# A fused attention, gated feed-forward and token/channel mixing kernel: the first batch in three units of 192 tokens instead of two of 288

## The reference

```python
# 1: attention; heads 0-3 look at the last 32 keys, heads 4-7 at every 4th of the last 128
scores = where(mask, q @ k.T / 8, -1e9)          # softmax over keys, then @ v
x = attention.transpose(0, 2, 1, 3).reshape(4, 576, 512)
# 2: gated feed-forward with a shift by one token
xk = mu_k * x + (1 - mu_k) * x_prev;  xr = mu_r * x + (1 - mu_r) * x_prev
x = sigmoid(xr @ w_r) * (relu(xk @ w_k) ** 2 @ w_v)        # w_k 512x1024, w_v 1024x512
# 3: mixing
u = x + (relu(x.T @ w_tok1) @ w_tok2).T
out = u + relu(u @ w_ch1) @ w_ch2
```

## Time and profile before

| | |
|---|---|
| runs (3) | 782.77 us median, 782.66 to 783.21 |
| the profiled execution | 783.69 us, of which its span is 781.9 us |
| PE busy | 741.8 us, 95% of the span |
| DVE, ACT, POOL busy | 375.3, 256.7, 238.4 us |
| mean granted TensorE clock | 0.995 |

### The profile page before, as it was taken

How to read it: one execution, slowest core, us unless ns; L and a number is a source line. 1 busy time by engine, 2 the same in 40 slices (tenths; PEclk the granted TensorE clock), 3 DMA queues, 4 the chain that set the end, 5 groups by cost and what they waited for, 6 DMA issues and landing times.

```text
span 781.9 us, 15662 instructions
## 1 busy us (share of the span) xinstructions
PE 741.8 (95%) x6616; PEld 716.2 (92%) x6616; DVE 375.3 (48%) x594; ACT 256.7 (33%) x636; POOL 238.4 (30%) x245
## 2 busy tenths in 40 slices
PE   4778999999999999999999999999999999999997
PEld 3667999989898999989999999999999999999997
DVE  5737875757676675767674121521225111341211
ACT  2445354353535344353442111411123111241111
POOL 5848464564656455473407200000000000000000
PEclk9998999999999999999999999999999999999999
DMA  8912312302302212020180100210002100010001
GB/s 200 249 35 42 67 35 59 74 14 56 75 18 57 61 26 59 19 61 1 48 337 1 62 1 1 62 61 1 1 1 71 52 1 1 1 62 1 2 1 60
DMA packets 67797, 39.80 MB, mean 51 GB/s; under 512 B 55120, under 2 KB 59024, under 8 KB 67728
## 3 DMA queue, kind: packets, MB, share of 16 engines
q1 hardware_dynamic: 65583, 34.09, 16.7%
q0 software_dynamic: 1088, 4.72, 1.8%
q10 hardware_dynamic: 1056, 0.00, 0.1%
HBM read 29.36 MB, written 4.72 MB: 44 GB/s over the span
## 4 chain that ended last, share of the span: by engine, by line
PE 81%; POOL 8%; issue 3%; ACT 3%; DVE 3%; DMA 1%; ACTq 0%; DVEq 0%; SPq 0%; POOLq 0%
PE bank L605 13%; PE bank L606 12%; PE bank L607 12%; PE tq L605 5%; PE tq L606 5%; PE tq L607 5%; PE bank L529 3%; PE bank L1021 3%; PE bank L1020 3%; PE s L1021 3%; PE bank L1019 3%; PE s L1019 3%; PE s L1020 3%; PE bank L500 3%; PE s L425 2%
## 5 line engine op out<-in xcount | busy, mean ns | idle before, releaser
L605 PE MATMUL bank<-xk_hi,WK_hi 128*128 128x288 f32 x256 | 81.0, 317 | 11.2 <-ACT kr L651 7.5
L605 PE MATMUL bank<-k_hi,WV_hi 128*128 128x288 f32 x256 | 78.4, 306 | 0.0
L995 DVE SCALAR_TENSOR_TENSOR h_lo<-tq,h_hi 128x288 fp32r<-128x288 f32 x48 | 22.0, 458 | 115.8 <-ACT h_hi L991 115.8
L995 DVE SCALAR_TENSOR_TENSOR h_lo<-bank,h_hi 128x288 fp32r<-128x288 f32 x48 | 22.0, 458 | 115.5 <-ACT h_hi L991 115.5
L669 POOL TENSOR_TENSOR k_lo<-kr,k_hi 128x288 fp32r<-128x288 f32 x64 | 56.7, 890 | 67.6 <-ACT k_hi L665 67.6
L606 PE MATMUL bank<-xk_hi,WK_lo 128*128 128x288 f32 x256 | 76.9, 300 | 0.0
L607 PE MATMUL bank<-xk_lo,WK_hi 128*128 128x288 f32 x256 | 76.6, 299 | 0.0
L606 PE MATMUL bank<-k_hi,WV_lo 128*128 128x288 f32 x256 | 75.7, 296 | 0.0
L607 PE MATMUL bank<-k_lo,WV_hi 128*128 128x288 f32 x256 | 75.5, 295 | 0.0
L655 DVE TENSOR_TENSOR kr<-kr 128x288 f32<-128x288 f32 x64 | 45.1, 705 | 41.8 <-ACT kr L651 41.1
L703 DVE RECIPROCAL rg<-rg 128x288 f32<-128x288 f32 x32 | 62.5, 1953 | 1.1
(11 more groups left out here) (142 smaller groups left out, 2220.5 us busy)
## 6 DMA issues: line engine op xcount, KB each, us to landing
C_raw<-in_moe_w_ch SPq DMA_DIRECT2D x6, 1024.0 KB, 11.1
qraw<-in_q SPq DMA_DIRECT2D x24, 192.0 KB, 3.4
kraw<-in_k SPq DMA_DIRECT2D x24, 192.0 KB, 4.1
xcur<-X POOLq DMA_DIRECT2D x4, 1152.0 KB, 6.4
out_x<-ost SPq DMA_DIRECT2D x16, 240.0 KB, 2.6
vt<-in_v SPq DMA_DIRECT2D x44, 80.0 KB, 2.5
vt<-in_v SPq DMA_DIRECT2D x8, 320.0 KB, 3.3
WK_raw<-in_moe_w_k SPq DMA_DIRECT2D x4, 512.0 KB, 5.6
```

Of the source, the lines that this page charges most:

```text
L605: e.matmul(out_ap, wh, xh, start=start and i == 0, stop=False)
L995: e.scalar_tensor_tensor(lo, ps, 0.0, hi.bitcast(F32), ALU.max, ALU.subtract).then_inc(Z.h2l_done, 1)
```

## The change

The feed-forward is cut into nine units listed in `FU`: three of 192 tokens for the first batch, then two of 288 for each other batch. The prologue runs only chunks 0 and 1; the first unit starts behind them, and chunks 2 to 23 are laid into slots by a table, `STARTS`. The rounding of w_k goes from DVE to ACT, the rest from POOL to DVE for six of its eight pieces. The first q and k are loaded in halves, k by ACT's queue; later q, k and v of the first batch are loaded ahead into parts of X that are not yet used (`spare`). The first p transposes use three banks, and chunk 1 a second `pT`. Fourteen matmuls of the identity matrix stand ahead of the first transposes (`warm_up`), and the table of the exponential is loaded early. Everywhere in the feed-forward, the square is now max(product, 0) * relu read from PSUM, and so the bank of an `up` product is free only when the square is done.

```diff
+FU = [(0, SU * j, SU) for j in range(NSU)] + [(b, HALF * h, HALF) for b in range(1, B) for h in range(2)]
+NU = len(FU)
...
+        pT1 = at("pT1", [P, 4 * SU], F32, rg_offset)
...
-            def vector(e):
+            def scalar(e):
                 e.wait_ge(wk_in[i // 2], 16)
-                e.tensor_copy(hi, raw).then_inc(Z.wk_hi, 1)
+                e.activation(hi, raw, ACT.Copy).then_inc(Z.wk_hi, 1)
+
+            def vector(e):
+                e.wait_ge(Z.wk_hi, i + 1)
+                e.tensor_tensor(lo, raw, hi.bitcast(F32), ALU.subtract).then_inc(Z.wk_lo, 1)
 
             def gpsimd(e):
                 e.wait_ge(Z.wk_hi, i + 1)
-                e.tensor_tensor(lo, raw, hi.bitcast(F32), ALU.subtract).then_inc(Z.wk_lo, 1)
-            return dict(vector=vector, gpsimd=gpsimd)
+                e.tensor_tensor(lo, raw, hi.bitcast(F32), ALU.subtract).then_inc(Z.wk_lo_last, 1)
+            return dict(scalar=scalar, vector=vector) if i < 6 else dict(scalar=scalar, gpsimd=gpsimd)
...
+        def raw_q(s, u):
+            return spare(slice(0, 2 * QB), 3, u) if s == 1 else qraw[0:2 * QB, DM * u:DM * (u + 1)]
+
+        def raw_k(s, u):
+            return spare(slice(0, 2 * QB), 3, 2 + u) if s == 1 else kraw[0:2 * QB, DM * u:DM * (u + 1)]
...
+        def raw_v(n, rows, h, heads=1):
+
+            if n in (2, 3):
+                return spare(rows, 2, 2 * (n - 2) + h // 2)[:, 256 * (h % 2):256 * (h % 2 + heads)]
+            return vts[n % 2][rows, 256 * h:256 * (h + heads)]
...
+        def load_first(half):
+
+            h0 = 4 * half
+
+            def sync(e):
+                for u in range(2):
+                    load_rows(e, q, 0, raw_q(0, u), u, h0, 4, (Z.q_in_a, Z.q_in_b)[half])
+
+            def scalar(e):
+                for u in range(2):
+                    load_rows(e, k, 0, raw_k(0, u), u, h0, 4, (Z.k_in_a, Z.k_in_b)[half])
+            return dict(sync=sync, scalar=scalar)
...
+        def p_bank(n, h):
+
+            return (p_ps, mlp_ps[1], mlp_ps[0], p_ps)[2 * n + h] if n < 2 else p_ps
+
+        def p_buffer(n):
+            return pT1 if n == 1 else pT
...
         def difference(hh, d):
-            b, h = divmod(hh, 2)
-            f0 = HALF * h
+            b, t0, n = FU[hh]
 
             def gpsimd(e):
-                e.wait_ge(Z.x_done, 2 * (NSU * b + h + 1) + d // 2 + 1)
+                e.wait_ge(Z.x_done, 2 * (NSU * b + (t0 + n - 1) // SU) + d // 2 + 1)
                 wait(e, Z.xm_done, 2 * DT * (hh - 1) + DT + d + 1)
-                e.tensor_tensor(dif[:, HALF * d:HALF * (d + 1)], xcols(b, d, f0 + 1, HALF), xcols(b, d, f0, HALF), ALU.subtract)\
-                    .then_inc(Z.dif_done, 1)
+                e.tensor_tensor(tile(dif, d, n), xcols(b, d, t0 + 1, n), xcols(b, d, t0, n), ALU.subtract).then_inc(Z.dif_done, 1)
...
-                e.wait_ge(Z.relu_done, FT1 * hh + n + 1)
+                e.wait_ge(Z.sq_done, FT1 * hh + n + 1)
...
-                e.tensor_tensor(t, t, t, ALU.mult).then_inc(Z.sq_done, 1)
+                e.scalar_tensor_tensor(t, ps, 0.0, t, ALU.max, ALU.mult).then_inc(Z.sq_done, 1)
...
-        NHH = 2 * B
-        AHEAD = 4
+        STARTS = [-1, 4, 11, 18, 25, 31, 38, 45, 52, 60, 66, 72, 77, 83, 91, 98, 104, 110, 116, 122, 131, 139]
...
+        def warm_up():
+
+            def tensor(e):
+                for _ in range(14):
+                    e.matmul(mlp_ps[0][:, 0:P], ident[:, :], ident[:, :], start=True, stop=True)
+            return dict(tensor=tensor)
...
-            steps = loads() + [transposes(0), evictions(0), scores(0)]
-            for n in range(AHEAD + 1):
-                more, run_, old = n + 1 < AHEAD, n < AHEAD, 1 <= n <= AHEAD
-                steps += [transposes(n + 1)] if more else []
-                steps += [mask_max(n)] if run_ else []
-                steps += [p_transpose(n - 1, 0)] if old else []
-                steps += [evictions(n + 1)] if more else []
-                steps += [subtract_max(n)] if run_ else []
-                steps += [p_evict(n - 1, 0), p_transpose(n - 1, 1)] if old else []
-                steps += [split_wk(2 * n), split_wk(2 * n + 1)] if run_ else []
-                steps += [exponentials(n)] if run_ else []
-                steps += [p_evict(n - 1, 1)] if old else []
-                steps += [scores(n + 1)] if more else []
-                steps += [weighted_values(n - 1), x_evict(n - 1)] if old else []
-                if n == AHEAD - 1:
-                    steps += [difference(0, 0), difference(0, 1)]
-                steps += [sums(n), normalise(n)] if run_ else []
-                if n == AHEAD - 1:
-                    steps += [split_wr(0), split_wr(1)]
-                    steps += [mix(0, 0, 0), mix(0, 0, 1), mix_parts(0, 0, 0), mix_parts(0, 0, 1)]
-            return steps + [difference(0, 2), difference(0, 3), mix(0, 0, 2), mix(0, 0, 3), mix_parts(0, 0, 2), mix_parts(0, 0, 3)]
+            return loads() + [warm_up(), transposes(0), evictions(0), scores(0), mask_max(0), transposes(1), evictions(1), scores(1),
+                              subtract_max(0), exponentials(0), split_wk(0), split_wk(1), split_wk(2), split_wk(3),
+                              mask_max(1), sums(0), subtract_max(1), exponentials(1), normalise(0), split_wk(4), split_wk(5),
+                              sums(1), normalise(1), p_transpose(0, 0), p_transpose(0, 1), p_evict(0, 0), p_evict(0, 1),
+                              p_transpose(1, 0), weighted_values(0), p_evict(1, 0), p_transpose(1, 1), p_evict(1, 1),
+                              split_wk(6), split_wk(7), x_evict(0), weighted_values(1), transposes(2),
+                              difference(0, 0), mix(0, 0, 0), mix_parts(0, 0, 0), difference(0, 1), mix(0, 0, 1), mix_parts(0, 0, 1),
+                              x_evict(1), difference(0, 2), difference(0, 3), mix(0, 0, 2), mix_parts(0, 0, 2),
+                              mix(0, 0, 3), mix_parts(0, 0, 3)]
...
-            steps = [load_qk(0), load_v(0), load_v(1), load_weights1(w_k, WK, 0, 1, wk_in[0]), load_qk(1),
-                     load_weights1(w_k, WK, 1, 1, wk_in[1]), load_weights1(w_k, WK, 2, 1, wk_in[2]),
-                     load_weights1(w_k, WK, 3, 1, wk_in[3]), load_weights1(w_r, WR, 0, 4, Z.wr_in), load_v(2),
-                     load_weights1(w_v, WV, 0, 4, wv_in[0]), load_weights1(w_v, WV, 4, 4, wv_in[1]), load_v(3), load_qk(2)]
-            for n in range(AHEAD, ND):
+            steps = [load_first(0), load_table(), load_first(1), load_weights1(w_k, WK, 0, 1, wk_in[0], "scalar"),
+                     load_weights1(w_k, WK, 1, 1, wk_in[1], "scalar"), load_mu(), load_v(0), load_v(1),
+                     load_weights1(w_k, WK, 2, 1, wk_in[2]), load_weights1(w_k, WK, 3, 1, wk_in[3]), load_qk(1),
+                     load_weights1(w_r, WR, 0, 4, Z.wr_in), load_v(2), load_v(3),
+                     load_weights1(w_v, WV, 0, 4, wv_in[0]), load_weights1(w_v, WV, 4, 4, wv_in[1]), load_qk(2)]
+            for n in range(4, ND):
...
-            return 5 * (n - AHEAD) if n <= 9 else 25 + 20 * (n - 9) // 3
...
-            for n in range(AHEAD, ND):
-                t = slot(n)
-                late[t].append(transposes(n))
+            early = [[] for _ in range(UNITS * NU)]
+            main_ = [[] for _ in range(UNITS * NU)]
+            late = [[] for _ in range(UNITS * NU)]
+            for n, t in enumerate(STARTS, 2):
+                if t >= 0:
+                    late[t].append(transposes(n))
...
-            late[0].append(split_wr(2))
-            late[1].append(split_wr(3))
             for i in range(8):
-                late[2 + i].append(split_wv(i))
+                late[3 + i].append(split_wv(i))
...
-            e.wait_ge(Z.const_done, 9)
-            e.wait_ge(Z.zeroed, 1)
+            e.wait_ge(Z.const_done, 3)
```

More of the change, by code:

```diff
@@ new lines, in k_landed, with v_landed @@
+        def k_landed(n):
+            return ((Z.k_in_a, 32), (Z.k_in_b, 32), (Z.k_in_1, 32), (Z.k_in_1, 32))[n] if n < 4 else (Z.k_in, 32 * (n // 2 - 1))
+        def raw_v(n, rows, h, heads=1):
+            if n in (2, 3):
+                return spare(rows, 2, 2 * (n - 2) + h // 2)[:, 256 * (h % 2):256 * (h % 2 + heads)]
+            return vts[n % 2][rows, 256 * h:256 * (h + heads)]
+        def v_landed(n):
+            if n in (2, 3):
+                return (Z.v_in_2, Z.v_in_3)[n - 2], 16 * v_loads(n)
+            return v_in[n % 2], 16 * sum(v_loads(m) for m in range(n % 2, n + 1, 2) if m not in (2, 3))
@@ L359, in load_v @@
             return dict(sync=sync)
-        def v_landed(n):
-            return 16 * sum(v_loads(m) for m in range(n % 2, n + 1, 2))
         def transposes(n):
@@ L683, in ready @@
                         e.wait_ge(Z.wr_lo, kt + 1)
-                product(e, ps, WR, cols(DM, P * d, P), xr, cols(HALF, 0, HALF), range(DT),
-                        before=None if d else ready).then_inc(Z.mm_done, 1)
```

(7 more changed lines are left out.)

212 lines of the change are left out of this document (120 added, 92 removed).

## The result

The changed kernel takes 808.61 us (median of 4 runs, 808.39 to 810.07), the kernel before 782.71 beside it (782.50 to 783.21). The ratio is 1.033, interval 1.032 to 1.035: 26 us slower, where 4.5 faster was forecast. The profiled execution has a span of 806.6 us.

The account below looks back on a forecast made before the run. PE was taken as the bound from 49 us on, after a start set by chains across four engines. Terms -9.0, +2.6, +6.1, +0.1, -4.3 sum to -4.5: 782.77 becomes 778.3 us, range 770 to 787.

Parts of the forecast that it names:

- Losses in the first batch: PE's lost time in the first batch's three 192-token units: 11.1 us against 11.0 before, so +0.1; called the softest term.
- the first unit starves: Slower rival: ACT and DVE make the first three units lose 19 us, low clock costs 8 more; 786.3 us, chance 0.20.
- My walk: Slot-by-slot estimate of the first batch: first unit loses 8.7 us, second and third 1.2 each at the boundary.
- Columns: Price of the first batch's 720 products at 192 columns: 66.6 us instead of 64.0, so +2.6.
- The line through 288 and 512 columns: Matmul start distances at those two widths, read as a line, gave 0.0925 us for 192 columns.
- the bound from the 96-column transposes at 0.082: Lower bound for a 192-column matmul: not below 0.082 us, where the transposes run.
- the weight load bounds 192 columns: Slower rival: load and matmul cannot go below 0.107 us, 720 products take 77.0, +10.4; 788.7 us, chance 0.04.
- Start of the first unit: Chain ahead of the first feed-forward product: last input complete at 40.1 us instead of 49.15, gain -9.0.
- the walk of the start: Step-by-step timing of the prologue's chain across the engines, from the warm-up's end at 7.2 us to 40.1.
- Five pairs of waits: PE's waits for relu and POOL's softmax after the first batch: -8.2 + 2.9 + 1.0 = -4.3 us.
- -8.2: Removal of PE's five relu and five softmax waits from 146.95 to 364 us, as chunks meet units elsewhere.
- The hold: Bank kept until the square: 1.3 us more at the one remaining wait site, 1.0 allowed for smaller holds.

## Why the prediction was wrong

**The step that failed first is "Losses in the first batch", +0.1.** Measured they are +10.5, and where PE's products have the forecast's length (ten of twelve) the loss is 126.4 us from the last input (38.9) to 165.3, less 66.9 and 28.9: 30.6 against 11.0, +19.6. This is the rival "the first unit starves", with its 19 us of loss and the clock down in the gaps, to which I gave 0.20 and 786.3. It is the right mechanism with the wrong place and size: all three short units have it. My walk gave the second and third 32 to 33 us each, with 1.2 of loss; they took 41.12 and 42.44. I had argued from DVE's 24 us of work in 33, a busy share, where a chain decides. Of the 8 to 10 us more, 4.6 in each unit are the floor of the matmuls (240 x 0.019), the rest lost time. The timeline of the changed kernel at the second unit's wait shows the chain (the lines of PE are left out; it waited from 94.67 to 96.61):

```profile
92.58 1.25 POOL L516 TENSOR_TENSOR sm<-sm,stat 128x640 f32<-128x640 f32 x1
...
92.71 1.33 DVE L645 SCALAR_TENSOR_TENSOR mixed<-dif,mus,X 128x192 f32<-128x192 f32 x1
...
93.86 0.74 ACT L525 ACTIVATE sm<-sm 128x640 f32<-128x640 f32 x1 [1.51 <-POOL sm L516]
...
94.63 0.82 DVE L533 TENSOR_REDUCE stat<-sm 128x8 f32<-128x640 f32 x1 [0.59 <-ACT sm L525]
...
95.49 0.61 DVE L535 TENSOR_SCALAR stat<-stat 128x8 f32<-128x8 f32 x1
...
96.13 0.20 DVE L537 RECIPROCAL stat<-stat 128x8 f32<-128x8 f32 x1
96.25 0.31 DVE L730 SCALAR_TENSOR_TENSOR kr<-bank,kr 128x192 f32<-128x192 f32 x1
```

ACT waits for POOL's subtraction, DVE for ACT's exponential, the square (96.25) behind the chunk's sums, and PE for the square's bank until 96.61: from the subtraction to PE's start 4.0 us, nearly all of it work of the chunk (128x640, and the small results of its sums), which does not shrink with the unit. The same chain stands ahead of the waits that end at 137.74 and, with pieces of w_r and w_v between, at 54.59. A product of 12 matmuls is 12 x 0.1115 = 1.3 us here, 1.6 with 288 columns. The chain is as long as before, and the work that could cover it is shorter.

That the chain as a whole is the cause, and not one link, is the reading that the runs leave; it is not shown. Neither the products' length, nor the held bank, nor the places alone gave back more than 5.5 us, but that is also what one sees when two limits stand side by side and only one is taken away. The reverse, the chains made shorter with all matmuls kept, was not run, nor the clock held up inside the units. Which link would have to go was not found.

**Columns, +2.6.** This step failed as well. Measured +16.2, for the pair of load and matmul has a floor of 0.111 us. The line through 288 and 512 columns, and the bound from the 96-column transposes at 0.082, were both wrong; a row of another form of instruction was taken as a bound for this one. The rival "the weight load bounds 192 columns" had the fact and 0.04 as its chance. By the prediction's own sum this miss alone would have made 778.3 + 13.6 = 791.9. Taken out by itself it is worth less: leaving out 13.4 us of matmuls gave 3.5 us in the changed kernel and 5.5 with four chunks ahead, since waits and the low clock took the rest.

**Start of the first unit, -9.0.** Right in place, 38.65 us for 40.1; it was 1.4 better. It brings 1.8 us (808.12 to 806.33, both with even places), because the first batch then carries about 1.7 chunks more, near 6 us by the sum, and PE waits longer in it. That the unit begins at 1.2 GHz is no difference: it does so in the kernel before as well. **Fourteen identity products**: I counted them only in the walk of the start; they cost 2.3 to 2.6 us.

**Five pairs of waits, -4.3.** The step "-8.2" rested on the chunks' places, and these alone gave +1.3 in the kernel before, though more than half of the waits went. The hold, put down with 1.3 + 1.0, costs 4.9; the square, of which the prediction counted nothing because PE is the bound, gives 7.6. The two together gave -2.6 in the kernel before. That has the sign of the prediction's term and is luck: it comes from a part counted at nothing. In the changed kernel the stretch behind the first batch is 2.4 us longer, although PE waits less in it (4.6 us from 169.35 to 388, where the kernel before had 8.4 from 147 to 364; none of them for the relu or POOL's softmax); its low stretch at 170 us costs 3.4.

**The parts together**, by medians: other edits +0.9 (the square's gain among them), the identity products +2.6, the cut into three +21.5, the early start -1.8, the changed kernel's places +2.3: 25.5 of 25.9 (the medians of the kernel before beside these runs differ by 0.5). Of what would show it wrong, the prediction named starts 0.1 or more apart and a first unit over 45 us; both came (0.11, and 46.3). Of what would show it right, only the waits behind the first batch came.

## What to carry to other kernels

When a unit of PE's work is made shorter, ask which chains on the other engines keep their length (here a chunk's softmax, 4 us from subtraction to square) and count their crossings with PE for each unit, instead of adding up busy shares. To learn whether a term of a sum is a cause, leave that much work out and time it: 13.4 us of matmuls were worth 3.5. If little comes back, another limit stands beside it, and both have to be left out together before either is called the small one. Try an edit of a large change by itself: the square from PSUM, with its held bank, gained 2.6 us alone and 4.1 with the gaps ahead of the first unit filled.
